# Opening of an attention kernel: rows loaded once and doubled on chip, centroid norms in a chain of their own, similarities in three parts

## The chip, the core and the metric

One core of a Trainium2 chip runs the whole program. Its engines work side by side, each through its own list of instructions in order, and wait for each other through semaphores: TensorE (PE in the rows; PEld is its weight load), VectorE (DVE), ScalarE (ACT), GpSimd (POOL), and SyncE (SP), which here only issues DMAs. ScalarE issues a few as well. The metric is the device time of one execution in microseconds; lower is better.

## What is computed

Three layers in a row on float32 data: an attention that is masked by cluster, a mixture of eight experts with a hard choice, and a second mixture whose gates are balanced over eight rounds. The change touches the beginning of the first.

```python
# q, k, v: (2, 8, 768, 64); centroids: (8, 16, 64)
q_n = q / (np.linalg.norm(q, axis=-1, keepdims=True) + 1e-06)      # k_n, c_n in the same way
q_assign = np.argmax(np.einsum('bhsd,hcd->bhsc', q_n, c_n), axis=-1)   # k_assign from k_n
mask = q_assign[:, :, :, None] == k_assign[:, :, None, :]
scores = np.where(mask, scale * np.matmul(q, k.transpose(0, 1, 3, 2)), -1e9)
attn = softmax(scores)
attn_out = np.matmul(attn, v)
# then: experts (embeddings normalised, tau, w1, w2), then the second mixture
```

## The kernel before

Attention goes through 16 heads (2 batches times 8) of 768 tokens. A head's tokens are six tiles of 128. The steady loop takes one query tile in each step: TensorE computes its scores against all 768 keys (`scores`), VectorE adds the mask and takes the row maximum (`mask`, then `maxima`, L685 and L697), ScalarE takes the exponential (`exps`, L564), TensorE transposes the probabilities (`transpose_probs`, L428), ScalarE and VectorE split them into a high and a low part (L570, L643), and TensorE multiplies them by the values. The scores of a tile are issued three steps ahead.

Before a head can enter that loop it goes through `prep`. Its query and key rows are loaded with the 64 columns written twice, side by side, so that one 128x128 transpose gives the values on both halves of the partitions (`QR`, `KR`; 192 KB for each of the two copies). TensorE transposes them in three groups of four tiles (stages 0, 1 and 2: four query tiles; two query and two key tiles; four key tiles; L343). ScalarE writes the rounded high parts (`HI`, L549 and L551; semaphore `prep_hi`), VectorE the low parts (L643 for queries, L655 for keys; semaphore `prep_lo`). From them come the similarities to 16 centroids (`similarities`, two 16-column matmuls for each of 12 tiles, L369 to L373), the cluster number of each token (L665 to L676, then `IDB`, L770), and a row of key cluster numbers spread over all partitions (`key_ids`, L379, copied by ScalarE at L559). The mask compares the two.

In steady state `prep` of the next heads is woven into the steps. The first two heads (0 and 1) have nothing ahead of them, so their `prep` is written out by hand ahead of the loop, and this opening is what the change rewrites. No scheduler is involved: the order in each engine's function is the order in which it runs. What sets the order there before:

- SyncE (L315 to L320) issues head 0's query rows twice, its key rows twice, its values once, then the same five loads of head 1. ScalarE's queue issues the centroids, the expert embeddings and tau.
- `UnitRows` normalises the centroids and the eight expert embeddings together: VectorE sums the squares of both (L157, L159), ScalarE takes one root (L149), VectorE refines both in six small dependent instructions (`newton`, L174 to L184) and writes the unit centroids at once (L169), and the unit embeddings later (L169 again).
- TensorE fills gaps with matmuls on ones whose result nobody reads (`warm`, L492; 8, 4 and 6 of them, `WARM`).
- TensorE transposes head 0, then the unit centroids (L504). ScalarE splits the centroids into `CH` and `CHL` (L608, L609) after its last high part of head 0, VectorE into `CL` and `CHL` (L643) after its last low part.
- TensorE then runs head 0's 24 similarity matmuls, head 1's 12 transposes, the scores of tile 0, the key ids, the scores of tile 1, the query half of head 1's similarities, the transposes of the unit embeddings (L525), and the scores of tile 2. Step 0 follows with the transposes of tile 0's probabilities (L428).
- VectorE, before `maxima` of tile 2, waits for the transposed embeddings (`experts_t`), scales them by 1/tau into `fold` (L784) and frees the bank `ps_o`.

## Time and profile before

| | us |
|---|---|
| median of 3 runs | 1591.67 |
| lowest and highest of them | 1590.71, 1593.67 |
| profiled execution, whole time | 1594.29 |
| its span in the trace | 1592.5 |
| TensorE busy in the span | 1568.3 (98%) |
| VectorE, ScalarE, GpSimd busy | 1190.0, 770.6, 263.7 |

The trace starts at 0, and all moments below are microseconds from there. The opening is everything up to the first `maxima` at 20.16; attention runs to about 300, the two mixtures fill the rest. A row of the timeline gives the start, the duration, the engine, the line in the kernel, the operation and the tiles that it writes and reads; in brackets stands how long the engine was idle ahead of it and who ended that. A row of the view by stretches gives the busy time of each engine within the stretch with its count of instructions, and the clock that TensorE was granted as a share of 2.4 GHz: 1.00 is 2.4 GHz, 0.50 is 1.2 GHz.

### The profile page before, as it was taken

What the parts mean: (1) busy time and instruction counts of PE and PEld (TensorE: products, weight loads), DVE (VectorE), ACT (ScalarE), POOL (GpSimd) and SP (SyncE); (2) the same over time, 40 slices, a digit from 0 to 9 for tenths busy, and PEclk for the clock granted to TensorE, in tenths of its full rate; (3) what the DMA queues carried; (4) which work ended last, traced back from release to release, by engine and by line L of the source; (5) the groups of instructions that cost most, each with busy time, mean ns of one, the idle gap of its engine ahead of it and who ended that gap; (6) DMA issues with size and microseconds to landing.
All of it is one profiled execution on the core that took longest, in us unless ns stands there. A gap on an engine that the chain in (4) does not pass through costs nothing.

```text
span 1592.5 us, 27473 instructions
## 1 busy us (share of the span) xinstructions
PE 1568.3 (98%) x8404; PEld 1390.7 (87%) x8404; DVE 1190.0 (75%) x2026; ACT 770.6 (48%) x1418; POOL 263.7 (17%) x343
## 2 busy tenths in 40 slices
PE   8999999999999999999999999999999999999998
PEld 7999999778888788989999898989899998989897
DVE  7999999999999976876656666666656566666664
ACT  5777779888888852323232323233232333232321
POOL 2111111342333550000100100010001001100102
PEclk9999999999999999999999999999999999999999
DMA  4222323354344310100110010011001100100002
GB/s 101 61 60 69 79 59 90 86 198 148 143 151 151 106 41 27 40 28 27 47 33 27 29 51 27 27 40 40 27 27 45 35 27 28 52 26 27 27 0 79
DMA packets 123701, 94.92 MB, mean 60 GB/s; under 512 B 66345, under 2 KB 101161, under 8 KB 123633
## 3 DMA queue, kind: packets, MB, share of 16 engines
q1 hardware_dynamic: 120848, 86.01, 17.8%
q0 software_dynamic: 2480, 8.13, 1.5%
q8 instruction: 21, 0.34, 0.1%
q14 instruction: 48, 0.39, 0.1%
q10 hardware_dynamic: 304, 0.05, 0.0%
HBM read 87.88 MB, written 6.29 MB: 59 GB/s over the span
## 4 chain that ended last, share of the span: by engine, by line
PE 88%; DVE 7%; issue 3%; ACT 2%; DVEq 0%; DMA 0%; ACTq 0%; POOL 0%
PE moe_bank L1381 11%; PE moe_bank L1383 11%; PE moe_bank L1382 11%; PE moe_bank L1356 10%; PE moe_bank L1359 10%; PE moe_bank L1358 10%; PE attn_ps_out L447 3%; PE attn_ps_probs_t L428 2%; PE moe_bank L1316 2%; PE moe_bank L1318 2%; PE moe_bank L1317 2%; PE moe_bank L1299 2%; PE moe_bank L1301 2%; PE moe_bank L1300 2%; DVE attn_scores L697 1%
## 5 line engine op out<-in xcount | busy, mean ns | idle before, releaser
L2035 DVE SCALAR_TENSOR_TENSOR all_x<-moe_bank,all_x 128x512 f32<-128x512 f32 x336 | 251.4, 749 | 130.8 <-PE moe_bank L1383 130.2
L1356 PE MATMUL moe_bank<-moe_x_t_hi,all_w_hi 128*128 128x384 f32 x896 | 303.0, 338 | 2.0 <-DVE all_w_lo L889 1.4
L1359 PE MATMUL moe_bank<-moe_x_t_hi,all_w_lo 128*128 128x384 f32 x896 | 302.5, 338 | 0.0
L1381 PE MATMUL moe_bank<-moe_w_hi,moe_h_hi 128*128 128x512 f32 x768 | 302.3, 394 | 0.0
L1358 PE MATMUL moe_bank<-moe_x_t_lo,all_w_hi 128*128 128x384 f32 x896 | 301.1, 336 | 0.0
L1382 PE MATMUL moe_bank<-moe_w_lo,moe_h_hi 128*128 128x512 f32 x768 | 300.5, 391 | 0.0
L1383 PE MATMUL moe_bank<-moe_w_hi,moe_h_lo 128*128 128x512 f32 x672 | 264.5, 394 | 0.0
L1356 PEld LDWEIGHTS moe_bank<-moe_x_t_hi,all_w_hi 128*128 128x128 f32 x896 | 168.4, 188 | 13.4 <-issue 2.0
L1358 PEld LDWEIGHTS moe_bank<-moe_x_t_lo,all_w_hi 128*128 128x128 f32 x896 | 168.4, 188 | 10.0
L1359 PEld LDWEIGHTS moe_bank<-moe_x_t_hi,all_w_lo 128*128 128x128 f32 x896 | 168.2, 188 | 0.0
L2196 POOL TENSOR_TENSOR moe_w_sums<-moe_dense_w_raw 128x256 f32<-128x256 f32 x32 | 24.8, 774 | 842.4 <-DVE all_w_lo L889 842.4
L1382 PEld LDWEIGHTS moe_bank<-moe_w_lo,moe_h_hi 128*128 128x128 f32 x768 | 144.1, 188 | 23.0
L1381 PEld LDWEIGHTS moe_bank<-moe_w_hi,moe_h_hi 128*128 128x128 f32 x768 | 144.3, 188 | 21.5
L1383 PEld LDWEIGHTS moe_bank<-moe_w_hi,moe_h_lo 128*128 128x128 f32 x672 | 126.0, 188 | 30.1
L1729 ACT ACTIVATE moe_h_hi<-all_x 128x384 fp32r<-128x384 f32 x63 | 33.1, 525 | 170.4 <-DVE all_x L2147 170.4
L889 DVE TENSOR_TENSOR moe_routed_w_lo<-moe_w_raw,moe_routed_w_hi 128x1024 fp32r<-128x1024 f32 x76 | 112.8, 1524 | 0.1
L1705 ACT ACTIVATE moe_h_hi<-moe_p 128x384 fp32r<-128x384 f32 x63 | 33.1, 525 | 143.2 <-DVE moe_p L2101 143.2
L2101 DVE TENSOR_TENSOR moe_p<-moe_bank,moe_p 128x384 f32<-128x384 f32 x63 | 35.1, 557 | 86.8 <-PE moe_bank L1359 76.1
L643 DVE TENSOR_TENSOR attn_probs_t_lo<-attn_ps_probs_t,attn_probs_t_hi 128x384 fp32r<-128x384 f32 x192 | 97.3, 547 | 2.4 <-ACT attn_probs_t_hi L570 1.3
L1724 ACT ACTIVATE moe_h_hi<-moe_bank 128x384 fp32r<-128x384 f32 x63 | 31.0, 492 | 134.2 <-PE moe_bank L1359 134.2
L697 DVE CUSTOM_DVE_ANT_0 attn_scores<-attn_ps_scores,attn_mask 128x768 f32<-128x768 f32 x96 | 91.2, 950 | 2.5 <-issue 0.6
L564 ACT ACTIVATE attn_probs<-attn_scores,attn_row_max 128x768 f32<-128x768 f32 x96 | 91.4, 952 | 3.4 <-DVE attn_row_max L697 3.3
(339 smaller groups left out, 3071.4 us busy)
## 6 DMA issues: line engine op xcount, KB each, us to landing
all_w_raw<-in_moe_w SPq DMA_DIRECT2D x8, 2048.0 KB, 7.5
moe_w_raw<-in_moe_w SPq DMA_DIRECT2D x8, 2048.0 KB, 8.3
moe_dense_w_raw<-in_moe_w SPq DMA_DIRECT2D x64, 256.0 KB, 2.9
moe_dense_w_raw<-in_moe_w SPq DMA_DIRECT2D x32, 512.0 KB, 3.4
attn_q_raw<-in_q SPq DMA_DIRECT2D x32, 192.0 KB, 3.0
attn_k_raw<-in_k SPq DMA_DIRECT2D x32, 192.0 KB, 3.5
attn_v_raw<-in_v SPq DMA_DIRECT2D x16, 192.0 KB, 3.5
tokens<-all_x SPq DMA_DIRECT2D x32, 96.0 KB, 1.9
```

Source lines behind the costliest of these rows:

```text
L447: mm = pe.matmul(out, V2[j][:, m, :], probs[(s0 // 3) % 2][:, m, :], start=(m == 0 and probs is PTH), stop=(m == T - 1 and probs is PTL))
L564: act.activation(PR[s % 2][:], SM[s % 2][:], ACT.Exp, bias=MX[s % 2][:], scale=-1.0, accum_out=SUM[:, s % 12:s % 12 + 1]).then_inc(exp_don ...
L643: return dve.tensor_tensor(out, src, hi.bitcast(F32), ALU.subtract)
L697: dve.tensor_tensor_reduce(out=SM[s % 2][:].rearrange("p (a k) -> p a k", a=2), in0=ps_s[s % 2][:, :, 0:3 * P], in1=MASK[s % 2][:].rearran ...
L889: return dve.tensor_tensor(out, src, hi.bitcast(F32), ALU.subtract)
L1356: pe.matmul(out, hi[:, s, k, :], XH[chunk][:, x, k, :], start=(start and k == 0), stop=False, skip_group_check=True)
L1358: pe.matmul(out, hi[:, s, k, :], XL[chunk][:, x, k, :], start=False, stop=False, skip_group_check=True)
L1359: mm = pe.matmul(out, lo[:, s, k, :], XH[chunk][:, x, k, :], start=False, stop=(stop and k == 1), skip_group_check=True)
L1381: pe.matmul(out, HH[h][hidden][:, rows], W2H[j][:, f, :], start=(f == 0), stop=False)
L1382: pe.matmul(out, HH[h][hidden][:, rows], W2L[j][:, f, :], start=False, stop=False)
L1383: mm = pe.matmul(out, HL[h][hidden][:, rows], W2H[j][:, f, :], start=False, stop=(f == 1))
L2035: dve.scalar_tensor_tensor(acc, y, PROB[:, row, bass.ds(at, 1)], acc, ALU.mult, ALU.add).then_inc(y_added, 1)
```

## The change

What it does, engine by engine:

- **Loads.** The four loads of head 0's query and key rows become two, each into the first half only. VectorE copies the second half of the queries, ScalarE that of the keys. For head 1 also two of four loads go, and GpSimd makes both copies, ahead of its split of head 0's values. The expert embeddings and tau are now loaded from SyncE's queue.
- **Norms.** Centroids and embeddings have a chain each. The centroids' starts as soon as they are loaded. The embeddings' sums, and the writing of the unit embeddings, go to ScalarE, behind head 0's high parts; the second activation table load (for the exponential) moves to behind them. VectorE does the embeddings' six small steps ahead of head 0's cluster numbers.
- **Centroid split.** `CH`, `CHL`, `CL` now come ahead of the high and low parts of stages 1 and 2 where they used to come behind them.
- **Similarities of head 0** wait for the low parts of stages 0, 1 and 2 one after the other, four tiles each, no longer for all three at once.
- **TensorE's order behind them**: scores of tile 0, four transposes of head 1, two filler matmuls, the key ids, the other eight transposes, scores of tile 1, three fillers, scores of tile 2, four fillers, the query half of head 1's similarities, the embeddings.
- **VectorE's and ScalarE's order**: the splits of head 1's stages 1 and 2 move behind the key ids on ScalarE, and on VectorE behind `maxima` of tile 0 and of tile 1.

```diff
-WARM = (8, 4, 6)
+WARM = (7, 4, 2, 3, 4, 6)
@@ class UnitRows: one object now holds one array
-    def load(self, act):
-        for j, (rows, _) in enumerate(self.arrays):
-            act.dma_start(self.raw[j][:], rows).then_inc(self.loaded[j], 16)
+    def load(self, engine):
+        engine.dma_start(self.raw[:], self.rows).then_inc(self.loaded, 16)
+    def sums(self, dve):
+        dve.wait_ge(self.loaded, 16)
+        dve.tensor_tensor(self.square[:], self.raw[:], self.raw[:], ALU.mult).then_inc(self.squared, 1)
+        dve.wait_ge(self.squared, 1)
+        dve.tensor_reduce(self.s[0], self.square[:], AX.X, ALU.add).then_inc(self.summed, 1)
+    def sums_of_squares(self, act):
+        act.wait_ge(self.loaded, 16)
+        act.activation(self.square[:], self.raw[:], ACT.Square, accum_out=self.s[0]).then_inc(self.summed, 1)
+    def write_by_scalar(self, act):
+        act.wait_ge(self.step, self.SCALED)
+        for out, raw in self.outputs():
+            act.activation(out, raw, ACT.Copy, scale=self.s[2]).then_inc(self.written, 1)
...
@@ sync
-            for half in range(2):
-                sp.dma_start(QR[0][:, :, half, :], qd[0:1].rearrange("o p t d -> p (o t) d")).then_inc(first_q, 16)
-            for half in range(2):
-                sp.dma_start(KR[0][:, :, half, :], kd[0:1].rearrange("o p t d -> p (o t) d")).then_inc(first_k, 16)
+            sp.dma_start(QR[0][:, :, 0, :], qd[0:1].rearrange("o p t d -> p (o t) d")).then_inc(first_q, 16)
+            sp.dma_start(KR[0][:, :, 0, :], kd[0:1].rearrange("o p t d -> p (o t) d")).then_inc(first_k, 16)
             sp.dma_start(VR[0][:], vd[0:1].rearrange("o p t d -> p (o t) d")).then_inc(first_v, 16)
-            load(1, 1)
+            embeddings.load(sp)
...
@@ tensor
-            pe.wait_ge(prep_lo, 3)
-            similarities(0, 0, ps_o[:, P:P + 2 * T * NC], 0)
-            similarities(0, 0, ps_o[:, P:P + 2 * T * NC], T).then_inc(prep_ready, 1)
+            for first in range(0, 2 * T, 4):
+                pe.wait_ge(prep_lo, first // 4 + 1)
+                mm = similarities(0, 0, ps_o[:, P:P + 2 * T * NC], first, 4)
+            mm.then_inc(prep_ready, 1)
+            scores(0, 0, 0)
             pe.wait_ge(raw_loaded[1], LOADS)
             transpose_raw(1, 0, 4, ps_s[1][:, 0]).then_inc(prep_ready, 1)
-            transpose_raw(1, 4, 4, ps_s[1][:, 1]).then_inc(prep_ready, 1)
-            transpose_raw(1, 8, 4, ps_t[:, 1]).then_inc(prep_ready, 1)
-            scores(0, 0, 0)
+            warm(WARM[2], ps_s[1][:, 1])
             pe.wait_ge(idb_ready, 1)
             key_ids(ps_t[:, 0], 0)
             key_ids(ps_p[:], 3)
+            transpose_raw(1, 4, 4, ps_s[1][:, 1]).then_inc(prep_ready, 1)
+            transpose_raw(1, 8, 4, ps_t[:, 1]).then_inc(prep_ready, 1)
             pe.wait_ge(prep_lo, 5)
             scores(1, 1, 0)
+            warm(WARM[3], ps_o[:])
+            pe.wait_ge(max_done, 1)
+            scores(2, 2, 0)
+            warm(WARM[4], ps_o[:])
             pe.wait_ge(kid_ready, 2)
             pe.wait_ge(prep_lo, 6)
             similarities(1, 1, ps_p[:], 0)
...
-            pe.wait_ge(max_done, 1)
-            scores(2, 2, 0)
@@ scalar
+            cents.load(act)
+            cents.roots(act)
+            act.wait_ge(first_k, 16)
+            act.activation(KR[0][:, :, 1, :], KR[0][:, :, 0, :], ACT.Copy).then_inc(first_k2, 1)
             prep(0, 0, 0)
             prep(0, 0, 1, ps_t[:, 0])
-            prep(0, 0, 2, ps_t[:, 1])
             act.wait_ge(cent_ready, 1)
             act.activation(CH[:], ps_o[:, 0:P], ACT.Copy).then_inc(cent_split, 1)
             act.activation(CHL[:], ps_o[:, 0:P], ACT.Copy).then_inc(cent_split, 1)
+            prep(0, 0, 2, ps_t[:, 1])
+            embeddings.sums_of_squares(act)
+            embeddings.roots(act)
+            act.wait_ge(made, 4)
+            act.activation(TABLE[:], c["rank16"][:, 0:1], ACT.Exp)
+            embeddings.write_by_scalar(act)
...
@@ gpsimd
+            for raw, loaded in ((QR[1], second_q), (KR[1], second_k)):
+                pool.wait_ge(loaded, 16)
+                pool.tensor_copy(raw[:, :, 1, :], raw[:, :, 0, :]).then_inc(raw_loaded[1], 32)
             pool.wait_ge(first_v, 16)
             split_v(0, 0)
```

VectorE, splits of head 0 (stages by their tile: `attn_ps_prep` is stage 0, `attn_ps_probs_t` stages 1 and 2) and of the centroids, before:

```order
L169 TENSOR_SCALAR attn_unit_centroids<-attn_raw,attn_row_norms 128x64
L643 TENSOR_TENSOR attn_q_lo<-attn_ps_prep,attn_qk_hi 128x512 [waits attn_prep_hi]
L643 TENSOR_TENSOR attn_q_lo<-attn_ps_probs_t,attn_qk_hi 128x256 [waits attn_prep_hi]
L655 SCALAR_TENSOR_TENSOR attn_qk_hi<-attn_ps_probs_t,attn_qk_hi 64x256
L655 SCALAR_TENSOR_TENSOR attn_qk_hi<-attn_ps_probs_t,attn_qk_hi 64x512 [waits attn_prep_hi]
L643 TENSOR_TENSOR attn_c_lo<-attn_ps_out,attn_c_hi 128x128 [waits attn_cent_split]
L643 TENSOR_TENSOR attn_c_hi_over_lo<-attn_ps_out,attn_c_hi 64x128
```

and in the changed kernel:

```order
L171 TENSOR_SCALAR attn_unit_centroids<-attn_centroids_raw,attn_centroids_norms 128x64
L662 TENSOR_TENSOR attn_q_lo<-attn_ps_prep,attn_qk_hi 128x512 [waits attn_prep_hi]
L662 TENSOR_TENSOR attn_c_lo<-attn_ps_out,attn_c_hi 128x128 [waits attn_cent_split]
L662 TENSOR_TENSOR attn_c_hi_over_lo<-attn_ps_out,attn_c_hi 64x128
L662 TENSOR_TENSOR attn_q_lo<-attn_ps_probs_t,attn_qk_hi 128x256 [waits attn_prep_hi]
L674 SCALAR_TENSOR_TENSOR attn_qk_hi<-attn_ps_probs_t,attn_qk_hi 64x256
L674 SCALAR_TENSOR_TENSOR attn_qk_hi<-attn_ps_probs_t,attn_qk_hi 64x512 [waits attn_prep_hi]
```

The centroids' two instructions moved from behind three splits of stages 1 and 2 to ahead of them.

TensorE, from behind the last of head 0's similarities to the key ids (L379), before:

```order
L373 MATMUL attn_ps_out<-attn_c_lo,attn_qk_hi 128x16
L343 MATMUL attn_ps_scores<-all_ident,attn_q_raw 128x128 [waits attn_raw_loaded1]
L343 MATMUL attn_ps_scores<-all_ident,attn_q_raw 128x128 x5
L343 MATMUL attn_ps_scores<-all_ident,attn_k_raw 128x128 x2
L343 MATMUL attn_ps_probs_t<-all_ident,attn_k_raw 128x128 x4
L417 MATMUL attn_ps_scores<-attn_qk_hi 128x384
L418 MATMUL attn_ps_scores<-attn_qk_hi,attn_q_lo 128x384
L417 MATMUL attn_ps_scores<-attn_qk_hi 128x384
L418 MATMUL attn_ps_scores<-attn_qk_hi,attn_q_lo 128x384
L379 MATMUL attn_ps_probs_t<-all_identb,attn_key_id_b 128x128 [waits attn_key_id_b_ready]
L379 MATMUL attn_ps_probs_t<-all_identb,attn_key_id_b 128x128 x2
```

and in the changed kernel, where the key ids are L390:

```order
L428 MATMUL attn_ps_scores<-attn_qk_hi 128x384
L429 MATMUL attn_ps_scores<-attn_qk_hi,attn_q_lo 128x384
L428 MATMUL attn_ps_scores<-attn_qk_hi 128x384
L429 MATMUL attn_ps_scores<-attn_qk_hi,attn_q_lo 128x384
L354 MATMUL attn_ps_scores<-all_ident,attn_q_raw 128x128 [waits attn_raw_loaded1]
L354 MATMUL attn_ps_scores<-all_ident,attn_q_raw 128x128 x3
L503 MATMUL attn_ps_scores<-all_onesb 128x512 x2
L390 MATMUL attn_ps_probs_t<-all_identb,attn_key_id_b 128x128 [waits attn_key_id_b_ready]
L390 MATMUL attn_ps_probs_t<-all_identb,attn_key_id_b 128x128 x2
L390 MATMUL attn_ps_prep<-all_identb,attn_key_id_b 128x128 x3
L354 MATMUL attn_ps_scores<-all_ident,attn_q_raw 128x128 x2
L354 MATMUL attn_ps_scores<-all_ident,attn_k_raw 128x128 x2
```

Eight of the twelve transposes of head 1 moved from ahead of the key ids to behind them.

VectorE, from the splits of head 1 to `fold`, before (the ISA rows with `attn_scores` are `maxima`):

```order
L655 SCALAR_TENSOR_TENSOR attn_qk_hi<-attn_ps_scores,attn_qk_hi 64x256
L655 SCALAR_TENSOR_TENSOR attn_qk_hi<-attn_ps_probs_t,attn_qk_hi 64x512 [waits attn_prep_hi]
L169 TENSOR_SCALAR attn_unit_experts<-attn_raw,attn_row_norms 8x8x64 x2
L685 TENSOR_SCALAR attn_mask<-attn_key_id_rows,attn_cluster_id 128x768 [waits attn_kid_ready]
L697 ISA attn_scores,attn_row_max<-attn_ps_scores,attn_mask 128x768 [waits attn_scores_ready,attn_mask_ready]
L697 ISA attn_row_max 128x1
L685 TENSOR_SCALAR attn_mask<-attn_key_id_rows,attn_cluster_id 128x768
L697 ISA attn_scores,attn_row_max<-attn_ps_scores,attn_mask 128x768 [waits attn_scores_ready,attn_mask_ready]
L697 ISA attn_row_max 128x1
L685 TENSOR_SCALAR attn_mask<-attn_key_id_rows,attn_cluster_id 128x768 [waits attn_max_done]
L781 RECIPROCAL attn_tau<-attn_tau 128x1 [waits attn_tau_loaded]
L784 TENSOR_SCALAR all_fold<-attn_ps_out,attn_tau 128x8x8 [waits attn_experts_t,attn_tau_inverse]
```

and in the changed kernel:

```order
L704 TENSOR_SCALAR attn_mask<-attn_key_id_rows,attn_cluster_id 128x768 [waits attn_kid_ready]
L716 ISA attn_scores,attn_row_max<-attn_ps_scores,attn_mask 128x768 [waits attn_scores_ready,attn_mask_ready]
L716 ISA attn_row_max 128x1
L662 TENSOR_TENSOR attn_q_lo<-attn_ps_scores,attn_qk_hi 128x256 [waits attn_prep_hi]
L674 SCALAR_TENSOR_TENSOR attn_qk_hi<-attn_ps_scores,attn_qk_hi 64x256
L704 TENSOR_SCALAR attn_mask<-attn_key_id_rows,attn_cluster_id 128x768
L716 ISA attn_scores,attn_row_max<-attn_ps_scores,attn_mask 128x768 [waits attn_scores_ready,attn_mask_ready]
L716 ISA attn_row_max 128x1
L674 SCALAR_TENSOR_TENSOR attn_qk_hi<-attn_ps_probs_t,attn_qk_hi 64x512 [waits attn_prep_hi]
L704 TENSOR_SCALAR attn_mask<-attn_key_id_rows,attn_cluster_id 128x768 [waits attn_max_done]
L803 RECIPROCAL attn_tau<-attn_tau 128x1 [waits attn_tau_loaded]
L806 TENSOR_SCALAR all_fold<-attn_ps_out,attn_tau 128x8x8 [waits attn_experts_t,attn_tau_inverse]
```

The writes of the unit embeddings left this engine, and two splits of head 1 (queries of the second tile group, and keys) moved to between the maxima of tiles 0 and 1, one to behind the maxima of tile 1.

## Rows read from the trace of the kernel before

**Rows 1.** Stretches (busy time by engine, granted clock, DMA), opening and attention proper.

```profile
...
10.10:10.90 0.80, 0.76 (x7) 0.76 (x7) 0.00 (x0) 0.00 (x0) 0.00 (x0) 1.00 0.62 165
10.90:14.50 3.60, 3.60 (x19) 3.60 (x18) 0.00 (x0) 0.00 (x0) 0.00 (x0) 0.51 1.05 236
14.50:17.80 3.30, 3.30 (x15) 3.30 (x16) 2.73 (x8) 1.65 (x4) 0.00 (x0) 0.50 0.09 32
17.80:19.50 1.70, 1.67 (x14) 1.18 (x13) 1.67 (x4) 1.07 (x3) 0.00 (x0) 1.00 0.00 0
40.00:60.00 20.00, 19.80 (x142) 18.66 (x141) 19.80 (x50) 15.78 (x37) 2.28 (x4) 1.00 0.25 61
...
```

**Rows 2.** Timeline (start, duration, engine, line, operation), first 7 us.

```profile
...
0.79 1.37 SPq L316 DMA_DIRECT2D attn_q_raw<-in_q  x2
...
2.63 0.37 DVE L157 TENSOR_TENSOR attn_square<-attn_raw 128x64 f32<-128x64 f32 x1 [1.70 <-DMA attn_raw<-in_centroids]
...
5.13 0.20 ACT L149 ACTIVATE attn_row_norms<-attn_row_norms 128x2 f32<-128x2 f32 x1 [1.43 <-DVE attn_row_norms L159]
5.35 1.28 ACT L603 ACT_TABLE_LOAD   x1
...
5.47 0.63 PE L343 MATMUL attn_ps_prep<-all_ident,attn_q_raw 128*128 128x128 f32 x4 [0.86 <-POOL all_fold L123]
...
6.57 0.42 DVE L169 TENSOR_SCALAR attn_unit_centroids<-attn_raw,attn_row_norms 128x64 f32<-128x64 f32 x2
...
6.72 0.87 PE L343 MATMUL attn_ps_probs_t<-all_ident,attn_k_raw 128*128 128x128 f32 x6 [0.40 <-DMA attn_k_raw<-in_k]
...
```

**Rows 3.** Loads of the query rows, first 20 us: time from issue to landing.

```profile
...
DMA to landing us min/median/max: 3.1/3.4/3.8
...
```

**Rows 4.** Timeline, 6.7 to 10.1 us: splits of the first head and the centroids.

```profile
...
6.75 0.58 ACT L549 ACTIVATE attn_qk_hi<-attn_ps_prep 128x512 fp32r<-128x512 f32 x1
...
7.29 0.51 POOL L816 CAST attn_v_hilo<-attn_v_raw 128x384 fp32r<-128x384 f32 x1 [1.92 <-DMA attn_v_raw<-in_v]
...
7.54 1.03 PE L492 MATMUL attn_ps_scores<-all_onesb 128*128 128x512 bf16 x4
...
8.40 1.03 DVE L655 SCALAR_TENSOR_TENSOR attn_qk_hi<-attn_ps_probs_t,attn_qk_hi 64x256 fp32r<-64x256 f32 x2
...
9.79 0.29 DVE L643 TENSOR_TENSOR attn_c_hi_over_lo<-attn_ps_out,attn_c_hi 64x128 fp32r<-64x128 f32 x1
...
```

**Rows 5.** Timeline, 14.8 to 19.6 us: from similarities to the first mask.

```profile
...
14.81 0.36 DVE L665 TENSOR_REDUCE attn_sim_max<-attn_ps_out 128x12 f32<-128x192 f32 x1 [4.72 <-PE attn_ps_out L373]
...
16.37 0.17 DVE L770 CAST attn_key_id_b<-attn_cluster_id 128x6 bf16<-128x6 f32 x1
16.45 1.22 DVE L643 TENSOR_TENSOR attn_q_lo<-attn_ps_scores,attn_qk_hi 128x512 fp32r<-128x512 f32 x2
...
18.04 0.69 DVE L655 SCALAR_TENSOR_TENSOR attn_qk_hi<-attn_ps_probs_t,attn_qk_hi 64x512 fp32r<-64x512 f32 x1
...
18.17 0.34 PE L379 MATMUL attn_ps_probs_t<-all_identb,attn_key_id_b 128*128 128x128 bf16 x3
...
19.56 0.40 DVE L685 TENSOR_SCALAR attn_mask<-attn_key_id_rows,attn_cluster_id 128x768 bf16<-128x768 bf16 x1
...
```

**Rows 6.** Timeline, 20.1 to 25.4 us: the first tiles of attention.

```profile
...
20.16 0.96 DVE L697 CUSTOM_DVE_ANT_0 attn_scores<-attn_ps_scores,attn_mask 128x768 f32<-128x768 f32 x1 [0.20 <-DVE attn_mask L685]
...
20.91 0.66 PE L525 MATMUL attn_ps_out<-all_ident,attn_unit_experts 8*128 8x8 f32 x8
...
21.50 0.44 PE L417 MATMUL attn_ps_scores<-attn_qk_hi 128*128 128x384 f32 x1
...
22.30 0.82 PE L428 MATMUL attn_ps_probs_t<-all_ident,attn_probs 128*128 128x128 f32 x6
...
23.05 0.28 DVE L784 TENSOR_SCALAR all_fold<-attn_ps_out,attn_tau 128x64 f32<-128x64 f32 x1
...
25.35 0.92 PE L428 MATMUL attn_ps_probs_t<-all_ident,attn_probs 128*128 128x128 f32 x6 [0.30 <-DVE attn_probs_t_lo L643]
...
```

100 lines of the change are left out of this document (48 added, 52 removed).

## Prediction

> **What bounds the kernel now.** I read the view by stretches first. Once attention runs, TensorE is busy 19.80 of 20 us and VectorE as long [rows 1]: every step needs both, nothing there waits for a moment fixed by something else, so whatever the opening saves or loses goes one for one into the end, and nothing else in the program is touched. In the opening itself the same view shows TensorE's clock: 1.00 (2.4 GHz) up to 10.9, 0.50 (1.2 GHz) from there to 17.8, then 1.00 again [rows 1]. Seven 16-column matmuls took 0.76 us before the fall, 0.11 each; nineteen took 3.60 after it, 0.19 to 0.21 each. Before the fall TensorE had run four fillers to 8.57 and then stood until 10.1 [rows 4].
>
> Then the timeline, along the chain that sets the first maxima at 20.16: doubled key rows landed, transposes at 6.72 [rows 2]; splits, and behind them the centroids' split, its last piece at 9.79 to 10.08 [rows 4]; 24 similarity matmuls to 14.8; cluster numbers, 14.81 to 16.54; key ids only at 18.17, since TensorE was behind with twelve transposes and four scores at 1.2 GHz; mask at 19.56 [rows 5]; maxima at 20.16 [rows 6]. Behind that, the two moments that tell what attention gets: TensorE's first transposes of probabilities at 22.30, the second at 25.35, with 0.30 us of waiting ahead [rows 6].
>
> **Up to the similarities.** The first load of queries is issued at 0.79 in half of the pair's 1.37 [rows 2]. Loads of this kind landed 3.1 to 3.8 us after issue [rows 3]: 3.9 to 4.6; I take 3.9, since only the small loads are ahead of it. The trace has no doubling copy. On VectorE it lies between the 128-wide split (0.29) and the 512-wide one (0.69) [rows 4, 5], say 0.45; on ScalarE under the 512-wide one's 0.58; GpSimd's 384-wide cast took 0.51 [rows 4]. Queries doubled: 4.35, against transposes at 5.47 [rows 2]. Keys are issued 0.69 later: landed 4.6 to 5.3, say 5.0, doubled 5.5, against 6.72. The centroids, ready for their sums at 2.63, need no longer wait for the embeddings (root at 5.13) [rows 2]. But VectorE now stands at the queries until 4.35; then the small steps, 5.37 to 6.57 before, so 1.2, and the two writes, 0.42 [rows 2], give 6.0. TensorE takes 0.87 for the keys [rows 2] and 0.3 for the centroids: 6.7. ScalarE's two copies (about 0.5) and VectorE's two (0.6) now come directly: **7.85 instead of 10.08, 2.2 earlier.** The splits of stages 1 and 2 (1.4 to 1.5, of which 1.03 are the two in [rows 4]) end at 9.35. They lie beside the similarities, which ask for them at 8.8 and 9.7; if the thirds were not there they would cost 1.5.
>
> **Similarities to first maxima.** At 0.11 each, 24 take 2.7: VectorE reads them at 10.9 instead of 14.81, **3.9 earlier**. The embeddings' small steps (1.2) stand ahead of that on VectorE, 9.35 to 10.55, covered with 0.35 to spare. Cluster numbers take 16.54 - 14.81 = 1.7: 12.65. In that time TensorE has scores, four transposes and two fillers, about 1.7 from 10.7, so it is there. From key ids to maxima it took 20.16 - 18.17 = 2.0: **maxima at 14.65 instead of 20.16, 5.5 earlier.** ScalarE's work that moved in between (table load, two writes of at most 0.58, one split of 0.6) ends about 12.3, before the key rows at 13.1.
>
> **What is given back.** Now VectorE has splits of head 1 between its maxima, which before lay in its waiting time: from 14.65, 0.9 for maxima, two 256-wide splits of 0.4: 16.35. Only then may TensorE begin the scores of tile 1 (0.8 for four, 22.30 - 21.50 [rows 6]), since the bank held head 1's transposes. Three fillers (0.65; four took 1.03 with the last one's tail [rows 4]), scores of tile 2 (0.8), four fillers (0.85): 19.5. VectorE's next maxima (17.4 to 18.3) and its 0.69 split end at 19.0, so TensorE sets the pace. Twelve similarity matmuls (1.4) and the embeddings (22.30 - 21.50 is the scores, 21.50 - 20.91 = 0.6 these) follow: **the first probabilities are transposed at 21.5, against 22.30: 0.8 earlier.** VectorE, which before had the embeddings long ready, waits for them and scales at 21.6 against 23.05: 1.45 earlier. So the 0.30 that TensorE waited at 25.35 goes too: 24.25, **1.1 earlier**. Of 5.5 us, 4.4 are given back, 1.5 of them to moved splits and the rest to TensorE's serial run of fillers, similarities and embeddings ahead of the step's first work.
>
> **The clock.** The sum takes 2.4 GHz throughout. But behind its four fillers (to 7.3) the changed kernel again gives TensorE a short wait and then only 16-column matmuls, and these ran 3.60 us without bringing the clock back [rows 1]. If it falls at 11 as before, scores, four transposes and two fillers take 1.2 more, less 0.35 of slack: 0.85, and 0.25 remain of 1.1. I take the middle, 0.4: **0.7 earlier in all.** Where the clock falls later, the kernel before loses less too (up to about 1.9 of the twelve transposes and the similarities), so the difference can also be +1.2.
>
> **The number.** The profiled execution took 1594.29, of which 1592.5 is span; the sum there is 1594.29 - 0.7 = 1593.6. It lies 2.6 above the median, as its long stretch at 1.2 GHz may partly explain, so I put the difference to the median: 1591.67 - 0.7 = **1591.0**. The case's own range: -2.6 (loads at 3.1, clock up to the end) to +2.0 (slow loads 0.7 later, clock as above), 1589.1 to 1593.7.
>
> **A rule against it.** The second table load took 1.28 us and the root ahead of it ended at 5.33, the load starting at 5.35 [rows 2]; the split behind began at 6.75 [rows 4], so nothing beyond 1.28 shows. The Trainium skill, ScalarE: Activation LUTs, What ACT_TABLE_LOAD costs, gives each switch of set about 1.38 us of drain on top. By that rule the moved switch would push the key rows' copies back by 0.6 and the time would be 1591.6; by the row it is hidden.
>
> **Rivals.**
> - *The head start stays.* If TensorE's fillers, similarities and embeddings fit in waits that I have not seen, only the moved splits (1.5) are given back: 5.5 - 1.5 = 4.0, 1587.7. For it: TensorE then stands from about 14.0 to 16.4. Against it: the similarities of head 1 need the 0.69 split behind the second maxima, so they cannot use that time. 0.13.
> - *The clock falls a second time, slower.* TensorE is done with head 1's transposes at about 14.0 and stands to 16.4, 2.4 us, longer than the 1.5 ahead of the fall in [rows 1]. If 16.4 to 21.5 runs at 1.2 GHz, scores take 1.4 more, fillers 1.5, similarities 1.25, embeddings 0.2: 4.3, and with the 0.7 of the forecast +3.6: 1595.3. It decides from where about 0.8 of that price is paid. 0.12.
> - *The loads gain nothing.* Queries at 4.6 and keys at 5.3 or later push everything up to the maxima by 0.7; the run behind is serial from there, so 0.0: 1591.7. 0.05.
> - *The forecast*, 0.70.
>
> **How the numbers follow.** What a measurement of this kernel can tell from no change is about 0.2%, 3.2 us: below 1588.5 or above 1594.9. Faster has only the first rival (0.13), slower the second (0.12); forecast and third make 0.75 for within. To hold 8 in 10 the range reaches to the first rival's value and to about the second's: 1587.6 to 1595.0.
>
> **What would show it.** In the changed kernel's trace: key transposes near 5.5; the first similarity near 7.9; the first maxima near 14.6 (15.5 with the clock at 1.2 GHz from 11); the scores of tile 1 waiting for VectorE near 16.4; VectorE waiting for the embeddings until 21.6; first and second transposes of probabilities near 21.5 and 24.3. I am wrong if VectorE does not wait for the embeddings, or if the stretch from 16.4 to 21.5 has a clock of 0.50, or if the second transposes lie more than 3 us from 24.3.

## The result, and the profile after

| | before | after |
|---|---|---|
| median | 1591.91 (22 runs) | 1595.91 (22 runs) |
| lowest and highest | 1590.71, 1594.95 | 1594.42, 1597.10 |
| profiled execution, its span | 1594.29, 1592.5 | 1595.94, 1594.1 |

The ratio is 1.0019, with an interval of 1.0013 to 1.0024. The changed kernel is slower by 0.2%, and its median lies 0.9 us above the upper end of the forecast range. The quotient of the two medians would be 1.0025, that of the means 1.0022. Half of the runs of the kernel before lie between 1590.7 and 1591.7 and the other half between 1592.1 and 1595.0, so its median stands between two groups. The change costs 2 to 4 us, of which the ratio says 3.0.

All that follows goes by two moments: when VectorE begins the maxima of the first tiles, and how long attention takes from the maxima of tile 10 to those of tile 95. First the timeline of the changed kernel, TensorE (PE) and VectorE (DVE), up to the second transposes of probabilities. Columns: start, duration, engine, line, operation, and in brackets how long the engine had been idle and who ended that.

```profile
4.10 0.45 DVE L780 COPY attn_q_raw<-attn_q_raw 128x384 f32<-128x384 f32 x1 [1.06 <-DMA attn_q_raw<-in_q]
6.00 0.83 PE L354 MATMUL attn_ps_probs_t<-all_ident,attn_k_raw 128*128 128x128 f32 x6
8.14 0.28 PE L380 MATMUL attn_ps_out<-attn_c_hi_over_lo,attn_qk_hi 128*128 128x16 f32 x1 [0.33 <-DVE attn_c_hi_over_lo L662]
11.03 0.36 DVE L684 TENSOR_REDUCE attn_sim_max<-attn_ps_out 128x12 f32<-128x192 f32 x1 [0.36 <-PE attn_ps_out L384]
14.72 0.96 DVE L716 CUSTOM_DVE_ANT_0 attn_scores<-attn_ps_scores,attn_mask 128x768 f32<-128x768 f32 x1 [0.20 <-DVE attn_mask L704]
16.52 0.69 PE L428 MATMUL attn_ps_scores<-attn_qk_hi 128*128 128x384 f32 x1 [2.31 <-DVE attn_qk_hi L674]
18.47 0.96 DVE L716 CUSTOM_DVE_ANT_0 attn_scores<-attn_ps_scores,attn_mask 128x768 f32<-128x768 f32 x1 [1.55 <-PE attn_ps_scores L429]
22.95 0.87 PE L439 MATMUL attn_ps_probs_t<-all_ident,attn_probs 128*128 128x128 f32 x6
23.14 0.28 DVE L806 TENSOR_SCALAR all_fold<-attn_ps_out,attn_tau 128x64 f32<-128x64 f32 x1 [2.45 <-PE attn_ps_out L542]
25.62 0.87 PE L439 MATMUL attn_ps_probs_t<-all_ident,attn_probs 128*128 128x128 f32 x6
```

The first half is as forecast: keys transposed at 6.00 (6.72 in [rows 2]), similarities from 8.14 (10.14 in the kernel before), read by VectorE at 11.03 (14.81 in [rows 5]), first maxima at 14.72, which is 5.44 sooner than in [rows 6]. The second half is not. TensorE waits 2.31 us for VectorE; then VectorE waits 1.55 us for the scores of tile 1, and 2.45 us for the transposed embeddings. The transposes of probabilities start at 22.95 and 25.62, against 22.30 and 25.35 in [rows 6]: all of the head start and 0.3 to 0.7 us more are given back.

The view by stretches of the same kernel (stretch, its length, busy time with count of instructions for PE, PEld, DVE, ACT, POOL, granted clock, DMA share, GB/s):

```profile
8.20:11.00 2.80, 2.80 (x25) 2.80 (x26) 2.25 (x9) 2.28 (x6) 1.49 (x3) 1.00 0.00 0
14.20:16.20 2.00, 0.01 (x1) 0.00 (x0) 1.79 (x5) 1.39 (x4) 0.00 (x0) 1.00 0.65 169
16.30:19.60 3.30, 3.08 (x9) 2.13 (x10) 1.69 (x5) 0.58 (x3) 0.00 (x0) 0.50 0.00 0
19.70:23.00 3.30, 3.30 (x29) 2.73 (x27) 0.95 (x3) 0.80 (x2) 0.00 (x0) 1.00 0.02 5
```

The similarities ran at 2.4 GHz to the end. TensorE stood from 14.2 to 16.5, and right behind that the clock is 0.50 (1.2 GHz) to 19.6, where the scores of tiles 1 and 2 lie.

Then the loop. Maxima of tiles 10 and 95, in the kernel before and in the changed one:

```profile
45.61 0.95 DVE L697 CUSTOM_DVE_ANT_0 attn_scores<-attn_ps_scores,attn_mask 128x768 f32<-128x768 f32 x1
298.33 0.96 DVE L697 CUSTOM_DVE_ANT_0 attn_scores<-attn_ps_scores,attn_mask 128x768 f32<-128x768 f32 x1 [0.31 <-issue]
```

```profile
46.27 0.95 DVE L716 CUSTOM_DVE_ANT_0 attn_scores<-attn_ps_scores,attn_mask 128x768 f32<-128x768 f32 x1
300.02 0.96 DVE L716 CUSTOM_DVE_ANT_0 attn_scores<-attn_ps_scores,attn_mask 128x768 f32<-128x768 f32 x1 [0.31 <-issue]
```

That is 252.72 us before and 253.75 after: **the loop over heads, in which no line was changed, takes 1.03 us longer.** Below I call this distance the pace. Behind tile 95 the two traces stay 1.62 to 1.7 apart up to the end.

So the traces differ by 0.66 (opening) and 1.03 (loop), together 1.7, as 1595.94 - 1594.29 says. The medians differ by 4.0. The other 2.4 is the distance between the profiled execution of before and its median; that of after lies on its median.

### The profile page after: what moved, and what is told of

It is laid out like the page before. It is cut to its first block, busy times and chain, and to the rows that moved or that the text cites. A ratio compares the mean times of both kernels' runs of the same rounds, so it can differ in the third digit from the quotient of the medians.

```text
span 1594.1 us, 27497 instructions
## 1 busy us (share of the span) xinstructions
PE 1569.8 (98%) x8412; PEld 1389.2 (87%) x8412; DVE 1191.1 (75%) x2028; ACT 774.3 (49%) x1424; POOL 264.1 (17%) x345
## 4 chain that ended last, share of the span: by engine, by line
PE 83%; DVE 9%; issue 5%; ACT 2%; DVEq 1%; POOL 0%; DMA 0%; ACTq 0%; POOLq 0%
PE moe_bank L1406 11%; PE moe_bank L1408 11%; PE moe_bank L1407 11%; PE moe_bank L1381 10%; PE moe_bank L1384 10%; PE moe_bank L1383 10%; PE moe_bank L1341 2%; DVE attn_probs_t_lo L662 2%; PE moe_bank L1343 2%; PE moe_bank L1342 2%; DVE attn_scores L716 2%; PE moe_bank L1324 2%; PE moe_bank L1325 2%; PE moe_bank L1326 2%; PE attn_ps_out L458 2%
## 5 line engine op out<-in xcount | busy, mean ns | idle before, releaser
L1406 PEld LDWEIGHTS moe_bank<-moe_w_hi,moe_h_hi 128*128 128x128 f32 x768 | 144.3, 188 | 21.5
```

The costliest lines, as they stand in the source:

```text
L1406: pe.matmul(out, HH[h][hidden][:, rows], W2H[j][:, f, :], start=(f == 0), stop=False)
```

## The experiments

Each kernel was timed in five rounds beside the kernel before on the same chip. "Tile 0, 1, 2, 3" are the starts of maxima in the profiled execution, "low" is the length of the stretches before 32 us in which TensorE's clock was 0.50.

| kernel | tile 0, 1, 2, 3 | low, us | pace | ratio, 95% |
|---|---|---|---|---|
| before, first trace | 20.16 21.64 23.44 26.35 | 6.8 | 252.7 | 1 |
| e4_before | 18.75 20.23 22.02 24.93 | 3.4 | 252.8 | 1.0004 (0.9995, 1.0013) |
| after, first trace | 14.72 18.47 23.55 27.01 | 3.4 | 253.8 | 1.0019 (1.0013, 1.0024) |
| e12_after | 15.45 18.79 24.42 27.87 | 3.4 + 3.4 | 253.7 | 1.0015 (1.0006, 1.0024) |
| e1_fill | 15.17 18.30 22.74 26.20 | 3.4 | 253.7 | 1.0009 (1.0000, 1.0017) |
| e2_new_head_old_tail | 15.25 16.74 19.29 25.04 | 10.2 | 253.7 | 0.9988 (0.9979, 0.9997) |
| e3_old_head_new_tail | 18.99 22.08 26.52 29.56 | 6.8 | 252.8 | 1.0024 (1.0015, 1.0034) |
| e5_before_padded | 20.12 21.60 23.40 26.73 | 6.8 | 253.8 | 1.0008 (0.9999, 1.0017) |
| e6_after_padded | 17.24 20.31 24.75 27.77 | 6.8 | 253.2 | 1.0007 (0.9998, 1.0016) |
| e7_second_head_twice | 14.88 18.63 23.80 27.25 | 3.4 | 253.3 | 1.0012 (1.0003, 1.0021) |
| e8_no_serial_fillers | 15.05 18.76 23.20 28.01 | 3.4 + 6.8 | 253.6 | 1.0029 (1.0020, 1.0038) |
| e9_vector_order_back | 17.65 19.14 22.88 26.32 | 3.4 | 253.6 | 1.0013 (1.0003, 1.0022) |
| e10_old_order_place | 18.03 19.52 21.31 24.22 | 6.8 | 253.2 | 0.9987 (0.9978, 0.9996) |
| e11_old_order_fill | 16.16 17.64 19.44 22.35 | 3.4 | 253.1 | 0.9977 (0.9968, 0.9987) |
| e13_experts_first | 14.95 18.61 22.67 27.48 | 3.4 | 253.7 | 1.0015 (1.0006, 1.0024) |
| e14_experts_first_vector_order | 19.69 21.18 23.69 28.51 | 6.8 | 253.7 | 1.0001 (0.9992, 1.0010) |
| e15_before_filled | 18.47 19.95 21.75 26.87 | 10.2 | 252.7 | 0.9999 (0.9990, 1.0008) |

The pace falls into sharp groups and says something of the kernel. The opening of one trace says less: the same kernel has it 1.42 us apart in its two traces, with the clock low for 6.8 or 3.4 us. Where the two disagree, the ratio decides. Ratios with overlapping intervals are not told apart.

### Which half of the change loses

e2 keeps the loads, the norms and the thirds and puts back the old order behind the similarities; e3 is the kernel before with that order alone.

```diff
 # e2: TensorE, behind the similarities of head 0 (ScalarE, VectorE likewise)
-scores(0); transpose 0..3; fillers; key_ids; transpose 4..11
-scores(1); fillers; scores(2); fillers; similarities(1); experts
+transpose 0..11; scores(0); key_ids; scores(1)
+similarities(1); experts; scores(2)
```

> The changed kernel's loads, norms, centroid split and similarities by thirds, but behind the similarities the order of the kernel before on TensorE, ScalarE and VectorE (all twelve transposes of head 1 first, its splits ahead of the first mask, no extra fillers). Theory order: the head start is real (similarities end at 10.9) and is kept; first maxima near 15.5, first transposes of probabilities near 17.8, time 1587.5 to 1588.5. Theory loop: what costs is something in attention's steady loop that the change moved, whatever the order in the opening: 1589 to 1592. Theory that the head start is worth nothing: 1591.9.

> The kernel before with only the changed order behind the similarities (and its fillers: 2, 3, 4). Theory order: this part alone costs what was given back, some 3 to 5 us: first transposes of probabilities near 26, time 1595 to 1597. Theory loop or head: under 1 us, 1592 to 1593.

> The kernel before, unchanged, for a second trace: 1591.9. Theory clock: where the clock falls differs between executions, so the first maxima lie between 18.2 and 20.2 us. Theory loop: the twelve masks that are stretched to 1.05 to 1.2 us in its first trace are stretched by other amounts in this one; if they are the same to 0.02 us, the loop's pace is a property of the kernel.

e2 is faster than the kernel before (0.9988) although it has the slower loop; e3 is slower (1.0024) although it has the quick one. The new order behind the similarities is what loses. e10 below, which has e2's order, says the same on another chip (0.9987).

By its time e2 missed what I expected: 1587.5 to 1588.5, measured 1592.07. Five of its twelve runs lie at 1589.3 to 1589.7, six at 1593.0 to 1593.8, and its trace is one of the slow six: the clock is low for 10.2 us, the first transposes of probabilities come at 18.67 (17.8 expected), and at tile 3 nothing of the head start is left (25.04, against 24.93 in e4).

So openings are better compared in traces whose clock is low for as long. With 6.8 us of it, tile 3 of e3 comes 3.2 us behind that of the kernel before (29.56 and 26.35), that of e10 2.1 ahead (24.22). With 3.4 us, tile 3 of the changed kernel comes 2.1 behind e4 (27.01 and 24.93), that of e11, 2.6 ahead (22.35). e10 and e11 have the new head and the old order, with other loads of head 1 and three fillers in e11. Both ways, the head gains 2 to 3 us and the order loses more.

The stretch behind tile 0 shows how it loses: in e4 tile 2 comes 3.3 us behind tile 0, in e2 4.0, in e3 7.5 and in the changed kernel 8.8. In the old order the low parts of head 1 lie ahead of the first maxima, so that scores of tiles 0 and 1 are both ready for VectorE. In the new one scores wait for low parts, these for maxima, and the next maxima for the scores.

### Fillers and the clock

e1 puts ten fillers into TensorE's wait for the low part of tile 1; e8 takes away the seven that the change put into the serial run.

```diff
 # e1
+warm(10, ps_o[:])
 pe.wait_ge(prep_lo, 5)
 scores(1, 1, 0)
 # e8
-WARM = (7, 4, 2, 3, 4, 6)
+WARM = (7, 4, 2, 0, 0, 6)
```

> The changed kernel with ten more filler matmuls on TensorE ahead of its wait for the scores of tile 1 (where it stood from 14.2 to 16.5 us). Theory clock: the fall of the clock at 16.3 costs the changed kernel about 1.5 to 2 us, so with the wait filled the clock stays at 2.4 GHz, the first transposes of probabilities come at 21.5 instead of 22.95, and the time is 1594.3. Theory order: the serial run of TensorE behind the first maxima is what costs; the clock is secondary; then also about 1594.3, still above the kernel before by 2. Theory loop (the steady loop got slower): no change, 1595.9.

> The changed kernel without the two groups of three and four fillers on TensorE behind the scores of tiles 1 and 2 (they hold 1.50 us at the low clock and 1.04 at the full one in its trace). Theory order (the run maxima, low parts, scores, maxima of tiles 0 to 2 sets the opening; fillers lie in TensorE's waits): maxima of tile 3 at 26 to 27 as with them, ratio to the changed kernel within 0.0004. Theory fillers (they stand in the way of the second head's similarities and the scores of tile 2): 1.0 to 2.0 us sooner, ratio to the kernel before 1.0007 to 1.0015. Theory clock (they keep it up): later by 0.5 to 2, ratio 1.0025 or more.

e12 is the changed kernel again.

> The changed kernel, unchanged, as the measure for the three others on the same chip and as a second profiled execution of it: ratio 1.0019 to 1.0025; pace from tile 10 to tile 95 253.75 to 0.05 again; maxima of tile 3 at 26.5 to 28.5 us, by where the clock is low.

Stretches around that wait, e12 first, then e1:

```profile
11.50:14.50 3.00, 3.00 (x18) 2.29 (x16) 1.73 (x5) 1.92 (x5) 0.00 (x0) 0.53 0.92 203
15.00:17.60 2.60, 0.57 (x4) 0.36 (x3) 2.36 (x6) 1.99 (x5) 0.00 (x0) 1.00 0.41 96
17.70:21.00 3.30, 3.30 (x11) 2.04 (x11) 2.14 (x5) 1.03 (x2) 0.00 (x0) 0.51 0.00 0
```

```profile
11.60:14.60 3.00, 3.00 (x17) 2.37 (x17) 1.46 (x5) 1.56 (x4) 0.00 (x0) 0.52 1.15 238
14.80:16.90 2.10, 2.10 (x13) 1.05 (x11) 1.89 (x5) 1.82 (x4) 0.00 (x0) 1.00 0.39 93
17.00:21.00 4.00, 4.00 (x25) 2.83 (x24) 2.52 (x6) 1.23 (x4) 0.00 (x0) 1.00 0.00 0
```

Both had the clock low from about 11 to 14.5. In e12 TensorE was busy for 0.57 of the next 2.60 us, and the clock fell again at 17.7. In e1 it was busy throughout, and the clock stayed up. Tile 3 began 1.67 sooner, and the ratio is 1.0009 against 1.0019 and 1.0015 (1.0019 to 1.0025 was expected for e12). By the ratios the fall behind the wait costs 1.0 to 1.6 us (the intervals overlap, so that the ratios alone don't show it), and it is not all: with the wait filled the kernel is still no faster than before. The first transposes of probabilities came at 22.14 in e1, 0.6 later than expected.

The other traces say how far this goes. A wait of TensorE of 2.0 to 2.3 us lies there in five (the changed kernel, e12, e7, e8, e13), and in all five the clock falls within 0.6 us of its end. Shorter waits settle nothing. With the new head TensorE stands only 0.33 us ahead of the similarities, and yet the clock falls at 10 to 11 us in seven traces (e1, e6, e9, e10, e11, e12, e14) and not in the five others. In the wait for tile 1's low part, 0.76 and 0.83 us (e2, e15) have a fall 2.0 and 2.3 us behind them, and 1.02, 1.21 and 1.33 (e14, e9, e3) have none; nor have 1.56 us in e6, which has the changed kernel's order. Its stretches from there on:

```profile
17.00:18.50 1.50, 0.48 (x4) 0.24 (x2) 1.30 (x4) 1.38 (x4) 0.00 (x0) 0.96 0.00 0
18.50:21.00 2.50, 1.96 (x10) 1.55 (x11) 1.58 (x4) 0.77 (x2) 0.00 (x0) 1.00 0.00 0
21.00:27.00 6.00, 6.00 (x51) 5.20 (x50) 3.98 (x12) 2.93 (x6) 0.00 (x0) 1.00 0.02 4
```

e8 says that the seven fillers cost nothing. Tile 2 came 0.35 sooner without them, and then the clock fell once more:

```profile
20.00:24.00 4.00, 3.40 (x30) 3.39 (x31) 2.03 (x5) 1.61 (x4) 0.00 (x0) 0.93 0.02 4
24.00:31.00 7.00, 7.00 (x30) 5.63 (x28) 5.13 (x14) 3.09 (x7) 2.09 (x6) 0.53 0.00 1
```

Its ratio, 1.0029, is the highest of all. The interval (1.0020 to 1.0038) still touches those of the changed kernel, so that removing the fillers loses is likely and not shown; that it gains the 1.5 us that I had reckoned for them in the serial run is ruled out.

e15 asks whether the kernel before, too, has its low stretch from the 1.57 us in which TensorE stood.

```diff
-WARM = (8, 4, 6)
+WARM = (8, 12, 6)
```

> The kernel before with twelve fillers instead of four behind the centroids' transpose, so that TensorE has work in the 1.57 us ahead of the similarities where its trace shows it idle. Theory clock by idleness: the low level that begins at 11.0 or 12.4 us comes later or is shorter, maxima of tile 3 at 24 to 25 us, ratio 0.9990 to 0.9997. Theory that the opening's low level comes whatever lies there: tile 3 at 24.9 or 26.35 by its length as in the two traces of the kernel before, ratio 0.9998 to 1.0006.

```profile
8.60:10.10 1.50, 1.50 (x8) 0.50 (x6) 1.43 (x5) 0.34 (x2) 0.18 (x1) 1.00 1.05 256
10.20:18.50 8.30, 7.30 (x62) 6.95 (x62) 4.90 (x14) 2.51 (x6) 0.00 (x0) 1.00 0.51 126
18.70:28.40 9.70, 9.70 (x44) 9.40 (x44) 7.19 (x20) 5.24 (x11) 0.70 (x2) 0.50 0.00 1
```

The hole is filled, the similarities ran at 2.4 GHz, and then the clock was low for 10.2 us from 18.7 instead. The ratio is 0.9999, and tile 3 (26.87) fits neither of the times that I expected. Filling a hole moved the low stretch and did not remove it; how it comes about there, with TensorE busy for 7.30 of 8.30 us ahead and a wait of 0.83 us in it, stays open.

### Which engine's order

```diff
 # e9 and e14: VectorE
+prep(1,1,1); prep(1,1,2)
 mask(0,0,0); maxima(0,0)
-prep(1,1,1)
 mask(1,1,0); maxima(1,1)
-prep(1,1,2)
 # e13 and e14: TensorE
 warm(WARM[4], ps_o[:])
+the experts' transposes
 similarities(1, 1, ps_p[:], 0)
-the experts' transposes
```

> The changed kernel with VectorE's order alone put back behind the similarities: all three low parts of the second head ahead of the first mask and maxima; TensorE and ScalarE as changed. Theory VectorE's order: TensorE no longer waits until 16.5 us for the low part of tile 1 (it lies ahead of the first maxima, so near 15.2), maxima of tile 0 at 15.7 (14.7 in the changed kernel), of tile 1 at 17.2 (18.5), of tile 3 at 25.0 to 26.0 (27.0, where the clock is low for 3.4 us in both), ratio to the kernel before 1.0005 to 1.0014. Theory TensorE's order (its transposes behind the key ids and its fillers): maxima of tile 3 stays within 0.5 us of 27.0, ratio 1.0017 or more.

> The changed kernel with the eight small transposes of the unit experts moved ahead of the second head's similarities on TensorE (they stood behind them); all else as changed. In its two traces VectorE waits 2.45 and 3.00 us for them ahead of its fold constants, until 23.14 and 24.00. Theory TensorE's order: fold by 21.5, maxima of tile 2 at 21 to 22 (23.55, 24.42), maxima of tile 3 sooner by 0.5 to 1.5 than 27.0, then held by the second head's similarities; ratio 1.0008 to 1.0015. Theory that the maxima of tile 2 only wait, and those of tile 3 stand behind the similarities anyway: tile 3 within 0.3 of 27.0 to 27.9, ratio 1.0015 to 1.0022.

> The changed kernel with both: the experts' transposes ahead of the similarities on TensorE, and VectorE's order put back; what is left of the new order is TensorE's transposes behind the key ids, ScalarE's order and the fillers. Theory order by both engines: maxima of tile 0 at 17.0 to 17.7, of tiles 1 to 3 right behind each other as in the kernel before (3.3 us from tile 0 to tile 2, 6.2 to tile 3), tile 3 at 23.5 to 25.0, ratio 1.0000 to 1.0008. If it stays at 1.0013 the order of these two places isn't the cause.

Neither alone does much. e9 has tile 1 right behind tile 0, but tile 0 itself comes at 17.65 and not at 15.7 as I expected: on VectorE the low parts now stand ahead of it, and they wait for ScalarE, which still writes head 1's high parts behind the key ids. Then VectorE waits for the embeddings. Its timeline:

```profile
15.53 0.43 DVE L662 TENSOR_TENSOR attn_q_lo<-attn_ps_scores,attn_qk_hi 128x256 fp32r<-128x256 f32 x1 [1.57 <-ACT attn_qk_hi L566]
...
19.14 0.96 DVE L716 CUSTOM_DVE_ANT_0 attn_scores<-attn_ps_scores,attn_mask 128x768 f32<-128x768 f32 x1 [0.19 <-DVE attn_mask L704]
...
22.46 0.28 DVE L806 TENSOR_SCALAR all_fold<-attn_ps_out,attn_tau 128x64 f32<-128x64 f32 x1 [1.96 <-PE attn_ps_out L542]
```

e13 brings the embeddings, and tile 2, sooner by 0.9, and tile 3 stands behind the similarities of head 1 as before (27.48): my expectation of 0.5 to 1.5 sooner there was wrong. Together, in e14, tile 2 follows 4.0 us behind tile 0, and the ratio falls to 1.0001. Its trace does not show that gain: its profiled execution was the slowest of its eleven (1597.26; the clock was low for 6.8 us from about 10.3), tile 0 comes at 19.69 (17.0 to 17.7 expected) and tile 3 at 28.51 (23.5 to 25.0 expected), 8.8 us behind tile 0 where it is 6.2 in the kernel before. Between the two VectorE waits 0.72 us for the similarities of head 1, at full clock. The interval of e14 (0.9992 to 1.0010) overlaps those of e9 and e13. So "both engines' order" is likely by the ratio and not shown; how the loss divides between TensorE's, VectorE's and ScalarE's order I did not take apart.

### The loop

Two pauses are new in the loop, and no changed line is near them. GpSimd's cast ahead of its subtraction starts later behind the third of three copies, and VectorE pauses between reading out a tile and the maxima of tile 23. Of each kernel first GpSimd's third copy and cast in the step of tile 29, then VectorE's read-out and the maxima of tile 23. Before, changed, and e5:

```profile
99.76 0.24 POOL L842 CAST attn_cents_of_pair<-attn_c_lo 128x64 fp32r x1
99.98 0.50 POOL L816 CAST attn_v_hilo<-attn_v_raw 128x384 fp32r<-128x384 f32 x1
```

```profile
84.60 0.37 DVE L729 TENSOR_TENSOR all_x<-attn_ps_out,attn_denominator 128x216 f32 x1
84.89 0.94 DVE L697 CUSTOM_DVE_ANT_0 attn_scores<-attn_ps_scores,attn_mask 128x768 f32<-128x768 f32 x1
```

```profile
100.70 0.24 POOL L864 CAST attn_cents_of_pair<-attn_c_lo 128x64 fp32r x1
101.05 0.50 POOL L838 CAST attn_v_hilo<-attn_v_raw 128x384 fp32r<-128x384 f32 x1
```

```profile
85.25 0.37 DVE L748 TENSOR_TENSOR all_x<-attn_ps_out,attn_denominator 128x216 f32 x1
85.84 0.96 DVE L716 CUSTOM_DVE_ANT_0 attn_scores<-attn_ps_scores,attn_mask 128x768 f32<-128x768 f32 x1 [0.22 <-issue]
```

```profile
100.38 0.24 POOL L845 CAST attn_cents_of_pair<-attn_c_lo 128x64 fp32r x1
100.72 0.50 POOL L819 CAST attn_v_hilo<-attn_v_raw 128x384 fp32r<-128x384 f32 x1
```

```profile
84.93 0.36 DVE L730 TENSOR_TENSOR all_x<-attn_ps_out,attn_denominator 128x216 f32 x1
85.53 0.96 DVE L698 CUSTOM_DVE_ANT_0 attn_scores<-attn_ps_scores,attn_mask 128x768 f32<-128x768 f32 x1 [0.24 <-issue]
```

From copy to cast it is 0.22 before and 0.35 and 0.34 in the others; from read-out to maxima 0.29, 0.59 and 0.60. e5 is the kernel before with six instructions that count a semaphore which nobody reads, and nothing else:

```diff
 # e5 (before)                             # e6 (after): 6 and 4
+for _ in range(2): dve.sem_inc(pad_dve, 1)      # ahead of VectorE's first wait
+for _ in range(4): pool.sem_inc(pad_pool, 1)    # behind GpSimd's constants
```

> The kernel before, with six instructions more that only count a semaphore nobody reads: two on VectorE ahead of its first wait and four on GpSimd behind its constants, as many as the changed kernel has more on each engine ahead of the loop over heads. Measure: from the start of tile 10's maxima to that of tile 95's, 252.72 us in the kernel before, 253.75 in the changed one and in both kernels with its new head. Theory place (where the loop's instructions lie sets what the sequencers of GpSimd and VectorE lose in it): 253.7, the pauses of 0.1 on GpSimd ahead of its split and of 0.3 then 0.05 to 0.2 on VectorE between its reading of the output and the maxima of tiles 23, 35, 47 appear, ratio to the kernel before 1.0006. Theory data (what the new head loads and when, or the doubling, sets the pace): 252.7, ratio 1.0000.

> The changed kernel with ten such instructions more, six on VectorE and four on GpSimd, so that each has eight more ahead of the loop than the kernel before. Theory place with a repeat of eight: the loop goes back to 252.7 from 253.75 and the time falls by 1.0, to some 1.0013 of the kernel before. Place with a longer repeat: another pace, 252.7 to 254.5, but not needed to be 253.75 to 0.05. Theory data: 253.75 to 0.05, ratio as the changed kernel's, 1.0019 to 1.0025.

```diff
 # e7 (after)
-single loads of head 1's q and k; GpSimd waits for them and doubles them
+load(1, 1)      # both twice by SyncE, as before
```

> The changed kernel, with the second head's q and k loaded twice by SyncE as before, so that GpSimd has no doubling and none of its four instructions; all else as changed. Theory place: the pauses of 0.1 on GpSimd in every second head go (of the 1.03 that the loop adds some 0.65 belong to these), VectorE's stay: pace 253.1. Theory data by doubling on GpSimd: 252.7. Theory data by other loads: 253.75. Opening: the second head's loads end up to 3 us later (768 KB instead of 576 KB at 250 KB per us is 0.8 of it), so maxima of tile 3 within 1 us of the changed kernel's 27.0 at like clock.

**The pace depends on how many instructions stand ahead of the loop on GpSimd and VectorE.** e5 computes exactly what the kernel before computes, loads the same rows, and has the changed kernel's pace and both of its pauses. e7 takes GpSimd's four away and loses GpSimd's pause and about half of the 1.03 (253.3; I had expected 253.1). e6, with eight more than before on each, has neither pause, but a longer one elsewhere: VectorE's at tile 92 grows. That row in e10, where VectorE has as many and GpSimd none more, so that it is VectorE's:

```profile
288.35 0.36 DVE L744 TENSOR_TENSOR all_x<-attn_ps_out,attn_denominator 128x216 f32<-128x216 f32 x1
289.42 0.96 DVE L712 CUSTOM_DVE_ANT_0 attn_scores<-attn_ps_scores,attn_mask 128x768 f32<-128x768 f32 x1 [0.71 <-issue]
```

In the kernel before the idle time there is 0.29. Every kernel with the changed head, e6, e7, e10 and e11 apart, has 253.6 to 253.8; every one with the old head and no padding has 252.7 or 252.8. That the number of instructions does it is shown; by what mechanism is not. The Trainium skill, Advanced Engine Details and Errata, ISA Cache, says that an engine's instructions come in lines of 256, of which the store holds two; a line's end would then fall at another place of the loop when instructions are added ahead. The traces agree in that the first pause sits at a fixed count from the start in every kernel that has it (ahead of record 68 of GpSimd and record 319 of VectorE, counted with the semaphore and register records that the timeline leaves out), and is the longest (0.39 and 0.30 us more than in the kernel before, then 0.10 and 0.05 to 0.1). No run here measured the length of such a line, so this stays an explanation that fits.

GpSimd's 0.1 us reaches the end because VectorE's mask waits for it. Masks take 0.40 to 0.42 us [rows 5], but 12 of the 96 of the kernel before take 1.05 to 1.21 (11 of the changed kernel's up to 1.23), and every one of these ends 0.21 to 0.22 us behind GpSimd's subtraction beside it. The mask of tile 29, before and after:

```profile
100.67 1.12 DVE L685 TENSOR_SCALAR attn_mask<-attn_key_id_rows,attn_cluster_id 128x768 bf16<-128x768 bf16 x1
```

```profile
101.61 1.23 DVE L704 TENSOR_SCALAR attn_mask<-attn_key_id_rows,attn_cluster_id 128x768 bf16<-128x768 bf16 x1
```

The Trainium skill, Trainium Architecture — The Big Picture, What this means for kernel authors, calls the port that VectorE and GpSimd share an exclusive lock; these masks agree in that none is through before the subtraction. That a mask takes 0.6 to 0.8 us longer is no loss of that size: at tile 17 of the changed kernel the subtraction started 0.39 behind the mask, which then took 0.53, and the maxima of tile 18 still came 3.32 us behind those of tile 17, as before (3.33). VectorE stood 0.44 us ahead of its read-out there, and the view names no releaser.

### A version that beats both

```diff
 # e10: e2, with head 1 loaded twice by SyncE (e7), and
+for _ in range(6): dve.sem_inc(pad_dve, 1)
 # e11: e10, and on TensorE
 key_ids(ps_p[:], 3)
+warm(3, ps_o[:])
 pe.wait_ge(prep_lo, 5)
```

> Meant to beat both: the new head, the old order behind the similarities, the second head loaded twice by SyncE (GpSimd's instructions ahead of the loop are as many as before) and six counting instructions on VectorE (eight more than before). Theory place: pace from tile 10 to tile 95 252.7 to 253.2 instead of 253.74, so up to 1.0 us under the run with the new head and the old order (ratio 0.9988): ratio 0.9983, some 1589.3 to 1590.5. If the 0.41 us that the changed kernel with eight more on both engines lost at tile 92 belongs to VectorE, it is seen here again (pace 253.15); if to GpSimd, not (252.7). Theory that the earlier result was chance: ratio 0.9995 or more.

> The kernel of the run before this one and three fillers in TensorE's wait for the low parts of tile 1 (0.76 us idle there in the run with new head and old order). Theory clock: without that gap the low level that began at 16.3 us comes less often or is shorter, maxima of tile 3 at 22.5 to 24.5 us instead of 25.0, ratio lower by 0.0005 to 0.0015 than without the fillers. Theory that the gap is too short to matter: the same to 0.0004.

e10 has a pace of 253.2, 0.6 under e2's, so the loss at tile 92 is VectorE's; but its ratio (0.9987, 0.9983 expected) can't be told from e2's, and its time (1591.28) lies above the 1589.3 to 1590.5 that I expected. e11 is the fastest: 1590.18 against 1592.83 for the kernel before on the same chip, 0.9977. Its interval (0.9968 to 0.9987) lies clear of the kernel before and of the changed one, not of e10 and e2, so what its three fillers add is not shown. Its first tiles, VectorE:

```profile
16.16 0.96 DVE L713 CUSTOM_DVE_ANT_0 attn_scores<-attn_ps_scores,attn_mask 128x768 f32<-128x768 f32 x1 [0.20 <-DVE attn_mask L701]
...
17.64 0.96 DVE L713 CUSTOM_DVE_ANT_0 attn_scores<-attn_ps_scores,attn_mask 128x768 f32<-128x768 f32 x1 [0.19 <-DVE attn_mask L701]
...
19.44 0.96 DVE L713 CUSTOM_DVE_ANT_0 attn_scores<-attn_ps_scores,attn_mask 128x768 f32<-128x768 f32 x1
...
22.35 0.96 DVE L713 CUSTOM_DVE_ANT_0 attn_scores<-attn_ps_scores,attn_mask 128x768 f32<-128x768 f32 x1
```

Here the head start of 4.0 us over the kernel before's first trace at tile 0 is still 4.0 at tiles 1, 2 and 3. Against e4, where the clock was low as long, it is 2.6 throughout.

## Why the prediction was wrong

Three steps failed: the price of TensorE's run behind the first maxima, taken at 2.4 GHz throughout; "nothing else in the program is touched"; and the step from the profiled execution to the median. In the trace the forecast was 1593.6 and 1595.94 came: 1.36 us of that lie in the opening (0.66 later instead of 0.7 earlier) and 1.03 in the loop. The other 2.6 of the 4.9 us between forecast and median are the offset. The order of events was as forecast, and so was the way to the first maxima.

**The way to the first maxima** held: forecast 4.35, 5.5, 7.85, 10.9, 12.65 and 14.65 for queries, keys, similarities, reading, key ids and maxima; measured 4.55, 6.0 (key transposes), 8.14, 11.03, 12.82 and 14.72; e12, with the clock low from 11, had 15.45 where 15.5 was forecast for that case. The sum has 0.35 us without a source (24 similarities of 0.11 from 7.85 end at 10.5, not at 10.9). That the difference of 5.5 came out as 5.44 is luck in part: against e4 it is 4.0. Nothing beyond the 1.28 us of the table load showed there either: it ran from 8.74, and the exponential followed at 10.04.

**The order of the run behind them** held too: TensorE waited for VectorE to 16.52 (16.4), VectorE for the embeddings (to 23.14 instead of 21.6). What failed is its price. From the scores of tile 1 to the first transposes I had 5.1 us, all at 2.4 GHz; it took 6.43. The scores of tile 1, the three fillers and the scores of tile 2 took until 20.16 and should have taken until 18.7, as the clock was 0.50 from 16.3 to 19.6. So the transposes came at 22.95 and 25.62 instead of 21.5 and 24.25. A clock of 0.50 there was one of the prediction's own signs of being wrong.

**The rival that the clock falls a second time** was right in kind and place, and had 0.12. I had given it all of the stretch, 4.3 us; in the first trace the low clock covers 3.2 us of it and costs 1.3. In the rows that I had, a wait of 1.5 us of TensorE was followed by a fall; a wait of 2.4 us, which the change itself makes, deserved at least even chances. All five traces with a wait of 2.0 to 2.3 us have a fall there, and e1, which fills the wait, has none. That the measured median (1595.91) lies near this rival's 1595.3 is chance: most of the distance has the two causes below.

**"The forecast's clock term"** expected a fall at 11 as before. One trace of the changed kernel has it there (e12) and one does not, and the kernel before has 3.4 or 6.8 us of it. A single trace of the opening carries 1.4 us of chance.

**The offset to the median** is the largest miss. I saw that the profiled execution of before stood 2.6 over the median and ascribed that in part to its long low stretch, yet took a difference against that very stretch over to the median unchanged. For the changed kernel trace and median agree (1595.94 and 1595.91), for the kernel before they do not (1594.29 and 1591.91). So the base had 1.4 us in the opening that e4, the same kernel, does not have (1592.72 in all): against e4, tile 3 of the changed kernel comes 2.1 later, not 0.66. The last 0.8 to the median is not settled. A stretch at 1.2 GHz near 557 us, which the traces of before, after and e4 have and others don't (last section), would be of that size; and the median of the kernel before is itself loose, 1592.37 to 1592.99 in the four later sets of runs.

**"Nothing else in the program is touched"** was wrong by 1.03 us in the trace. I had priced the instructions that the change adds by their duration and cover, and not by what they do to the place of the loop behind them. e5 puts 1.0008 (0.9999 to 1.0017) on it, so the loop's loss is clear in the traces and not in the ratio.

The change laid against the runs, by their ratios, each good to about 1.4 us: place 1.03; new head with old order -1.9 in all (e2), so some -2.9 without the place; and the new order between +3.8 (e3) and +4.3 to 4.9 (changed kernel, 1.0015 and 1.0019, less e2). The sum with +4.3 to 4.9 is no test, as these were got from the changed kernel's own ratio; with e3's +3.8 it is one, and gives +1.9, within the intervals of the 2.4 and 3.0 measured. **The head start was worth 2 to 3 us and the order that was meant to use it cost more.**

## What to carry to other kernels

A head start passes on only if the work behind it keeps its slack: count, for the first two or three tiles, how far the last maxima trail the first (3.3 us in the old order, 8.8 in the new). When an edit makes TensorE wait for 2.0 to 2.3 us as here, price what follows at 1.2 GHz, or fill the wait. Before a difference is taken from a profiled execution over to the median, look at where that execution lies among the others: a second trace of the old kernel moved its opening by 1.42 us. And before a difference of 0.1% in a loop is explained by an edit elsewhere, add as many idle instructions to the old kernel and look whether the loop moves.

## What the runs showed of the hardware

- Six instructions ahead of a loop changed its time by 1.04 us in 253 (e5), and every kernel with the changed head and that number has 0.9 to 1.04 more; two on VectorE alone gave 253.3, eight on each 253.2.
- A bf16 mask on VectorE of 0.42 us takes up to 1.23 beside a subtraction on GpSimd and ends 0.21 to 0.22 behind it. One that started beside GpSimd's cast of 0.50 us took 0.53 (tile 17 of the changed kernel).
- Behind a wait of TensorE of 2.0 to 2.3 us the clock fell in five traces of five; at the same place it fell behind 0.76 and 0.83 us, and not behind 1.02 to 1.56 us (four traces).
- With TensorE busy for 7.30 of 8.30 us the clock could still fall, for 10.2 us (e15), and e2 had 10.2 us of it too. The same kernel can have 3.4 us or 6.8 us.
- Between the two mixtures, near 557 us, the clock is low for 3.4 us in nine of the traces and not in eight. The changed kernel has it in its first trace and not in e12. The way from tile 95 to the second mixture's first hidden layer took 274.3 to 274.6 us with it and 273.1 to 273.3 without.
